# One core, mLSTM and two expert layers: GpSimd's DMAs on two semaphores, an earlier first row load, another order of the weight split, the last block in halves

## The reference, cut to what matters

```python
# layer 1, expert e (exactly 384 tokens):
h = np.maximum(x[mask] @ w1[e], 0.0); out[mask] = h @ w2[e]        # 320 -> 1024 -> 320
# layer 2, expert e (as many tokens as chose it):
h = np.maximum(x[mask] @ w1[e], 0.0)
out[mask] = gate_w[mask, None] * (h @ w2[e])
```

## Time and profile before

| what | value |
|---|---|
| median of 3 runs | 801.45 us (800.43 to 802.65) |
| the profiled execution | 801.36 us, span 799.6 us |
| busy PE, DVE, ACT, POOL | 743.6, 433.1, 315.8, 407.8 us |
| TensorE clock granted, mean | 0.889 of full speed |
| chain that ended last | PE 60%, DVE 10%, POOL 10%, DMA 10%, issue 5%, ACT 2% |

### The profile page before, as it was taken

How to read it: one execution, slowest core, us unless ns; L and a number is a source line. 1 busy time by engine, 2 the same in 40 slices (tenths; PEclk the granted TensorE clock), 3 DMA queues, 4 the chain that set the end, 5 groups by cost and what they waited for, 6 DMA issues and landing times.

```text
span 799.6 us, 21236 instructions
## 1 busy us (share of the span) xinstructions
PE 743.6 (93%) x7388; PEld 649.0 (81%) x7395; DVE 433.1 (54%) x1243; ACT 315.8 (39%) x822; POOL 407.8 (51%) x557
## 2 busy tenths in 40 slices
PE   7999999898899988999999998799999999989992
PEld 3777778677777767999999997489899888979992
DVE  7898887666666674266666666633232332323221
ACT  3666666410000003567766677323233233323320
POOL 4677764700000017787878866507454474465530
PEclk9999999855555557999999999899999999999996
DMA  6666669526722203654644652456576866932310
GB/s 179 206 216 204 188 198 305 166 89 233 240 82 80 82 10 118 188 163 137 195 157 145 199 158 86 141 173 172 170 230 182 237 167 192 275 103 83 119 49 0
DMA packets 63587, 126.23 MB, mean 158 GB/s; under 512 B 14615, under 2 KB 46384, under 8 KB 61970
## 3 DMA queue, kind: packets, MB, share of 16 engines
q1 hardware_dynamic: 44770, 84.19, 33.8%
q0 software_dynamic: 6864, 29.92, 12.0%
q10 hardware_dynamic: 11872, 10.99, 5.2%
HBM read 93.58 MB, written 15.34 MB: 136 GB/s over the span
## 4 chain that ended last, share of the span: by engine, by line
PE 60%; DVE 10%; POOL 10%; DMA 10%; issue 5%; ACT 2%; SPq 0%; ACTq 0%; POOLq 0%
DMA w_hi<-w_raw 9%; PE bank L1662 8%; PE bank L1663 7%; PE bank L1664 7%; PE bank L1621 5%; POOL w_lo L878 3%; PE bank L1698 3%; POOL w_lo L845 3%; PE bank L1701 3%; PE bank L1702 3%; PE bank L1426 3%; PE bank L1499 2%; PE bank L1469 2%; PE bank L1597 2%; PE bank L1707 1%
## 5 line engine op out<-in xcount | busy, mean ns | idle before, releaser
L1662 PE MATMUL bank<-w_hi,hT_hi 128*128 (+1 forms) x440 | 141.3, 321 | 5.4 <-DVE hT_lo L1247 2.9
L1663 PE MATMUL bank<-w_lo,hT_hi 128*128 (+1 forms) x440 | 137.4, 312 | 0.0
L1664 PE MATMUL bank<-w_hi,hT_lo 128*128 (+1 forms) x440 | 137.1, 312 | 0.0
L878 POOL TENSOR_TENSOR w_lo<-w_raw,w_hi 128x320 fp32r<-128x320 f32 x128 | 109.7, 889 | 34.0 <-DMA w_hi<-w_raw 18.8
L845 POOL TENSOR_TENSOR w_lo<-w_raw,w_hi 128x256 fp32r<-128x256 f32 x128 | 95.2, 774 | 56.2 <-DMA w_hi<-w_raw 53.0
L818 POOL DMA_INDIRECT routing_arena<-x_rows,routing_arena x24 | 23.5, 979 | 151.5 <-DVE routing_arena L1235 142.4
L1662 PEld LDWEIGHTS bank<-w_hi,hT_hi 128*128 128x128 f32 x440 | 83.3, 189 | 8.0 <-issue 5.2
L1663 PEld LDWEIGHTS bank<-w_lo,hT_hi 128*128 128x128 f32 x440 | 83.3, 189 | 0.0
L1664 PEld LDWEIGHTS bank<-w_hi,hT_lo 128*128 128x128 f32 x440 | 83.4, 189 | 0.0
L1316 DVE TENSOR_TENSOR xT_lo<-bank,xT_hi 128x256 fp32r<-128x256 f32 x31 | 13.2, 425 | 110.1 <-ACT xT_hi L673 110.1
L687 ACT ACTIVATE hT_hi<-bank 128x512 fp32r<-128x512 f32 x62 | 33.7, 596 | 95.4 <-PE bank L1811 95.4
(11 more groups left out here) (290 smaller groups left out, 1807.4 us busy)
## 6 DMA issues: line engine op xcount, KB each, us to landing
w_raw<-in_moe_w SPq DMA_DIRECT2D x16, 1280.0 KB, 6.8
w_raw<-in_moe_w SPq DMA_DIRECT2D x16, 1024.0 KB
turn_arena<-in_moe_w2t SPq DMA_DIRECT2D x12, 768.0 KB, 4.9
w_raw<-in_moe_w SPq DMA_DIRECT2D x32, 256.0 KB
w_hi<-w_raw POOLq DMA_DIRECT2D x6, 1280.0 KB, 6.1
w_hi<-w_raw POOLq DMA_DIRECT2D x6, 1024.0 KB, 7.8
routing_arena<-x_sorted ACTq DMA_DIRECT2D x31, 160.0 KB
mlstm_arena<-in_q SPq DMA_DIRECT2D x32, 120.0 KB
```

Source lines behind the costliest of these rows:

```text
L878: last = nc.gpsimd.tensor_tensor(w2_part(w2_lo, n)[:, k, :], w2_raw[:, k, :], w2_part(w2_hi, n)[:, k, :], ALU.subtract)
L1662: T.matmul(dst, a_hi, b_hi, start=first, stop=False)
L1663: T.matmul(dst, a_hi, b_lo, start=False, stop=False)
L1664: return T.matmul(dst, a_lo, b_hi, start=False, stop=last)
```

## The change

It puts all DMAs of POOL on two semaphores, `landed_a` and `landed_b`, in place of nine. With one semaphore for several DMAs in flight a count tells which have landed only at the sum of all that were issued on it, so some waits are placed anew: the third gather of the first layer-1 expert is issued after the first has landed, and the output waits at every fourth block for all outputs before it (before, each waited for the one two before it). It makes the first two row loads of layer 2 depend on two numbers (`lead`) that DVE works out from expert 0's count, ahead of the tables; the first block's slot is fixed; 27 idle matmuls in place of 34. In `split_weights` the third slice of w1 is copied first and split first, then slices one and two, each with a DMA of its own, and w2's DMA is issued between the two. The second slice of expert 0's lo part is made by DVE in `logits_copies`. The last block's down product starts after half of its hidden values: PE turns the first half between the two halves of down(29), and down(30) goes to another bank.

```diff
-        scattered = sem("scattered")
+        landed_a, landed_b = sem("landed_a"), sem("landed_b")
-        hi1_ready, hi2_ready = sem("hi1_ready"), sem("hi2_ready")
-        rows_ready = sem("rows_ready")
-        rows_first = [sem(f"rows_first{b}") for b in range(BPE)]
-        stored = [sem(f"stored{s}") for s in range(2)]
...
+        A_FIRST, B_FIRST = 32, 16
+        A_SCATTERED = A_FIRST + 16 * G
+        B_ROWS = B_FIRST + 16 * (G - BPE)
+        A_WEIGHTS, B_WEIGHTS = 64, 16
+        B_STORED = B_ROWS + B_WEIGHTS * (E - RING)
...
-            def hidden_hi(i):
-                act.wait_ge(yb_ready, G + i + 1)
+            def hidden_hi(i, last=False):
                 for f in range(2):
+                    if last and f == 0:
+                        act.wait_ge(pe_made, PED["half_down"])
+                    elif last or f == 0:
+                        act.wait_ge(yb_ready, G + i + 1)
                     act.wait_ge(ht_ready, 2 * i + f + 1 + 2)
                     nc.scalar.activation(hT_hi[:, 4 * f:4 * f + 4, 0:128], bank[3 + f][:, :].rearrange("p (k t) -> p k t", k=4), ACT.Copy).then_inc(hh_ready, 1)
...
-                act.wait_ge(dve_made, DVED["first_rows"])
-                first = [act.value_load(tab2[0:1, 3, i:i + 1], min_val=0, max_val=E * REGION) for i in range(2)]
-
                 act.wait_ge(front_pads, 16 * (E + 1))
-                act.wait_ge(scattered, 16 * G)
+                first = []
+                for i in range(2):
+                    act.wait_ge(dve_made, DVED[f"lead{i}"])
+                    first.append(act.value_load(lead[0:1, i:i + 1], min_val=0, max_val=E * REGION))
+                act.wait_ge(landed_a, A_SCATTERED)
                 for i in range(2):
                     row_loads(first[i], i)
                 x_hi(0, 0)
+                act.wait_ge(dve_made, DVED["first_rows"])
                 next_rows(2, 0)
...
                 for b in range(BPE):
                     j = BPE * e + b
+                    if e == 0 and b == 2:
+                        pool.wait_ge(landed_a, 16)
                     pool.indirect_dma_start(rows[:, b, 0:KT * 128], None, x_sorted[:, :],
-                                            bass.IndirectOffsetOnAxis(ap=order[:, j:j + 1], axis=0)).then_inc(rows_ready if e else rows_first[b], 16)
-
-            def load_hi1(n):
-
-                s, m = n % RING, n - RING
-                pool.wait_ge(raw1_ready, 48 * (n + 1))
-
-                if m >= E:
-                    pool.wait_ge(slot1_free, m - E + 1)
-                pool.dma_start(w1_hi[:, s, 0:2, :], w1_raw[:, 0:2, :]).then_inc(hi1_ready, 16)
-                for h in range(2):
-                    pool.dma_start(w1_hi[64 * h:64 * h + LOW, s, 2, :], w1_raw[64:64 + LOW, 2, :]).then_inc(hi1_ready, 16)
+                                            bass.IndirectOffsetOnAxis(ap=order[:, j:j + 1], axis=0)).then_inc(landed_b if e or b == 1 else landed_a, 16)
 
             def make_lo1(n):
-                s, by_act = n % RING, n < E + RING
-                by_dma = n - E - RING
+                s = n % RING
                 if n:
                     pool.wait_ge(w2_ready, n)
-                if not by_act:
-                    pool.wait_ge(hi1_ready, 48 * (by_dma + 1))
-                for k in range(2):
+                for k in range(2 if n else 1):
                     for h in range(2):
-                        if by_act:
-                            pool.wait_ge(hi1_act, 2 * KT * n + 2 * k + h + 1)
-                        for q in range(2):
-                            c = slice(h * HF + q * HF // 2, h * HF + (q + 1) * HF // 2)
-                            last = nc.gpsimd.tensor_tensor(w1_lo[:, s, k, c], w1_raw[:, k, c], w1_hi[:, s, k, c], ALU.subtract)
-                if by_act:
-                    last.then_inc(w1_ready, 2)
-                    return
-                last.then_inc(w1_ready, 1)
-
-            def make_tail1(n):
+                        pool.wait_ge(hi1_act, 2 * KT * n + 2 * k + h + 1)
+                        last = lo1_half(s, k, h)
+                last.then_inc(w1_ready, 2 if n else 1)
+
+            def lo1_half(s, k, h):
+                for q in range(2):
+                    c = slice(h * HF + q * HF // 2, h * HF + (q + 1) * HF // 2)
+                    last = nc.gpsimd.tensor_tensor(w1_lo[:, s, k, c], w1_raw[:, k, c], w1_hi[:, s, k, c], ALU.subtract)
+                return last
+
+            def make_lo2(n):
                 s = n % RING
-                pool.wait_ge(w1_ready, 2 * n + 1)
-                pool.wait_ge(scattered, 16 * G)
-                pool.wait_ge(rows_ready, 16 * (G - BPE))
+                if n:
+                    pool.wait_ge(w1_ready, 2 * n + 2)
+                for k in range(FT):
+                    pool.wait_ge(hi2_act, FT * n + k + 1)
+                    last = lo2_part(n, k)
+                last.then_inc(w2_ready, 1)
+
+            def lo2_part(n, k):
+                return nc.gpsimd.tensor_tensor(w2_part(w2_lo, n)[:, k, :], w2_raw[:, k, :], w2_part(w2_hi, n)[:, k, :], ALU.subtract)
+
+            def split_weights(n):
+                s, m = n % RING, n - RING
+                at_a, at_b = A_SCATTERED + A_WEIGHTS * (m - E), B_ROWS + B_WEIGHTS * (m - E)
+                pool.wait_ge(raw1_ready, 48 * (n + 1))
+                pool.wait_ge(slot1_free, m - E + 1)
+                pool.wait_ge(w2_ready, n)
+                for h in range(2):
+                    pool.dma_start(w1_hi[64 * h:64 * h + LOW, s, 2, :], w1_raw[64:64 + LOW, 2, :]).then_inc(landed_a, 16)
+                pool.dma_start(w1_hi[:, s, 0, :], w1_raw[:, 0, :]).then_inc(landed_a, 16)
+                pool.dma_start(w1_hi[:, s, 1, :], w1_raw[:, 1, :]).then_inc(landed_b, 16)
+                pool.wait_ge(landed_a, at_a + 48)
                 for h in range(4):
                     c = slice(h * HF // 2, (h + 1) * HF // 2)
                     last = nc.gpsimd.tensor_tensor(w1_hi[64:128, s, 2, c], w1_raw[64:128, 2, c], w1_hi[64:128, s, 2, c], ALU.subtract)
                 last.then_inc(w1_ready, 1)
-
-            def load_hi2(n):
-                s, m = n % RING, n - RING
+                pool.wait_ge(w1_ready, 2 * n + 1)
+                for h in range(2):
+                    lo1_half(s, 0, h)
                 pool.wait_ge(raw2_ready, 16 * (n + 1))
-
-                if m >= E:
-                    pool.wait_ge(slot2_free, m - E + 1)
-                pool.dma_start(w2_part(w2_hi, n), w2_raw[:, :, :]).then_inc(hi2_ready, 16)
-
-            def make_lo2(n):
-                s, by_act = n % RING, n < E + RING
-                by_dma = n - E - RING
-                pool.wait_ge(w1_ready, 2 * n + 2)
-                if not by_act:
-                    pool.wait_ge(hi2_ready, 16 * (by_dma + 1))
+                pool.wait_ge(slot2_free, m - E + 1)
+                pool.dma_start(w2_part(w2_hi, n), w2_raw[:, :, :]).then_inc(landed_a, 16)
+                pool.wait_ge(landed_b, at_b + 16)
+                lo1_half(s, 1, 0)
+                lo1_half(s, 1, 1).then_inc(w1_ready, 1)
+                pool.wait_ge(landed_a, at_a + 64)
                 for k in range(FT):
-                    if by_act:
-                        pool.wait_ge(hi2_act, FT * n + k + 1)
-                    last = nc.gpsimd.tensor_tensor(w2_part(w2_lo, n)[:, k, :], w2_raw[:, k, :], w2_part(w2_hi, n)[:, k, :], ALU.subtract)
+                    last = lo2_part(n, k)
                 last.then_inc(w2_ready, 1)
 
...
+            pool.wait_ge(landed_a, A_SCATTERED)
+            pool.wait_ge(landed_b, B_ROWS)
             for n in range(E + RING, 2 * E):
                 split_weights(n)
...
-                if b > 1:
-                    pool.wait_ge(stored[b % 2], 16 * (b // 2))
+                if b and b % 4 == 0:
+                    pool.wait_ge(landed_b, B_STORED + 16 * b)
                 pool.indirect_dma_start(out, bass.IndirectOffsetOnAxis(ap=ids[:, b:b + 1], axis=0),
-                                        tokens[:, b, 0:DM], None, bounds_check=N - 1, oob_is_err=False).then_inc(stored[b % 2], 16)
-            for s in range(2):
-                pool.wait_ge(stored[s], 16 * ((NB2 + 1 - s) // 2))
+                                        tokens[:, b, 0:DM], None, bounds_check=N - 1, oob_is_err=False).then_inc(landed_b, 16)
+            pool.wait_ge(landed_b, B_STORED + 16 * NB2)
...
+                if g in (G - 6, G - 5):
+                    h = g - (G - 6)
+                    c = slice(h * HF, (h + 1) * HF)
+                    dve.wait_ge(hi1_act, 2 + h + 1)
+                    last = V.tensor_tensor(w1_lo[:, 0, 1, c], w1_raw[:, 1, c], w1_hi[:, 0, 1, c], ALU.subtract)
+                    if h:
+                        last.then_inc(w1_ready, 1)
...
+                done = bank[6 if isinstance(i, int) and i == NB2 - 1 else 5]
...
                         x_lo(i + 1, 1 - s)
+                    else:
+                        hidden_lo(i, (0,))
                     result(i - 1)
```

(49 more changed lines are left out.)

27 lines of the change are left out of this document (12 added, 15 removed).

## The result

The changed kernel took 794.07 us (median of 7, 793.05 to 795.99), the kernel before 801.79 us beside it on the same chip (median of 7, 798.2 to 805.11): ratio 0.9905, 95% interval 0.9879 to 0.993. That is a gain of 7.7 us where 15.3 had been forecast. The profiled execution took 794.07 us, with a span of 792.3 against 799.6. Single executions that came out some per cent longer at a lower granted clock, whatever the kernel, are left out of all ratios.

What follows compares the result with a forecast made beforehand. The prediction took PE to set the pace, POOL's weights nearly late in layer 2, and the span to end on POOL's DRAIN. Its six steps summed to -15.3 us: 801.4 to 786.1 us, whole range 783.8 to 793.5.

Steps and rivals of the forecast that it cites:

- Step 6: POOL's closing DRAIN of 8.48 us: seven semaphores fewer at 0.88 us each shorten it; -6.1 us, bounds 0 and -6.6.
- Rival (a): The closing DRAIN doesn't care about semaphores, being fixed or by DMAs issued; the rest holds, 792.2 us; chance 0.27.
- Step 1: Expert 0's second lo slice on DVE: first-phase `keys` lines run faster without POOL beside them; -1.2 us, bounds 0 and -1.6.
- Step 2: Layer 1's first expert: the third gather waits for the first to land; +0.7 us, bounds 0.3 and 1.2.
- Step 3: Start of layer 2: the first row loads go out earlier; -0.7 us, gain 0.4 to 1.4 or 0.
- Step 4: Layer 2's weight split: POOL's wait for w1's copies falls 2.1 us per turn, ending PE's stall at block 23; -4.6 us.
- Step 5: Last block in halves: no PE idle ahead of down(30), clock stays up; -3.4 us, bounds -1.8 and -3.6.

## Why the prediction was wrong, step by step

**Step 6, the DRAIN, failed: +0.5 us measured, -6.1 forecast.** The prediction read the right row, and said that what the DRAIN does isn't shown; then it chose the semaphores, "since no other row of the trace gives a reason" and since the number of DMAs "hardly changes". But the row and a count would have allowed both, and the second forecast was as easy: 103 DMAs make 8.4 us, and six more make 0.5 us more. One sample can't choose between two counts; the mistake was to put 6.1 us, the largest term of the sum, on that choice with a chance of 0.50 against 0.27. What the runs show in its place is 82 ns for each DMA since the last DRAIN, with two, three, nine or ten semaphores. The prediction had named this sign of being wrong itself: "if the DRAIN grew". Rival (a), in its form "by DMAs issued", is what happened: 792.2 us, plus 0.5 for six DMAs which it named and didn't price.

**The other steps** sum to -9.2 in the forecast. The trace has -9.8 from the logits to the last result, +0.6 of it in layer 1 in no step; then the mLSTM stage adds 2.1. That the two come so near is luck in part: 1.35 us of blocks 0 to 22 are not shown to be the change's, and some 1.5 us each at block 23 and at the last block were falls of the granted clock in the one trace of the kernel before.

- *Step 1*, -1.2 forecast, -1.6 + 0.45 found. `keys` gained all of its bound. The new pair on DVE cost the path nothing that shows, as costed; but DVE's own pair L1079 went from 1.96 to 2.50 us and its cover ran out (PE then waited 0.38 us). Its first instruction begins 0.17 us after one of GpSimd's now and takes 1229 ns; in the earlier trace rows it begins 0.01 us before one and takes 690. The Trainium skill (SBUF — State Buffer, Who interferes with whom) says that a DVE instruction with two SBUF inputs and a GpSimd one that reads SBUF shut each other out for a whole instruction. The trace agrees, for the pair that had not moved. Beside the new one (1082 and 671 ns) two of GpSimd's lo instructions took 1170 and 1306 ns in place of some 725.
- *Step 2*, +0.7 forecast, +0.8 found. *Step 3*, -0.7 forecast, -0.7 found to the first row load, and 0.35 more up to the first turn.
- *Step 4*, -4.6 forecast, -4.15 found at block 23. Each wait fell by 2.8 us (17.0 over six), not by 2.1, and w1 of n = 15 was whole at 704.1 (705 forecast). What the stall is worth differs between traces of the old split: 4.15 us here, with a wait of 2.53 us and a granted clock of 0.50 from 711.4 to 714.7 us behind it, and 1.3 us in the kernel before with three DRAINs, with a wait of 1.03 us and the clock at 1.00. The other 1.35 us, of blocks 0 to 22, are in no step and not shown to be the change's: that stretch took between 187.2 and 192.4 us in sixteen traces (190.3 before, 188.9 after), with no wait for weights above 0.3 us in it. By the Trainium skill (DMA: Bandwidth & Descriptors, Anatomy of one DMA) the bytes saved are worth an estimated 1.2 us per wait; the trace shows more than twice that. The prediction set all traced waits far above that rule's 5.6 us for the three copies; two of the six were 5.9 and 7.1 us.
- *Step 5*, -3.4 forecast, -3.5 found, of which about 1.5 is the clock. The prediction's bound of -1.8 was near the part that is sure (2.0), but for another reason: it let the clock fall in the changed kernel too, while in the runs it is the idle of 1.8 us that did not always bring a fall.
- *The start*, +2.1 us, was in no step, and is no effect of the change. Granted clock of PE, the first two stretches of 20 us, of before, of after and of the kernel with thirty DMAs (stretch, length, PE busy, PEclk, DMA share, GB/s):

```profile
0.00:20.00 20.00, 15.03 (x89) 1.00 0.63 179
20.00:40.00 20.00, 19.68 (x320) 1.00 0.66 206
```

```profile
0.00:20.00 20.00, 14.38 (x69) 0.91 0.61 174
20.00:40.00 20.00, 20.00 (x295) 1.00 0.63 194
```

```profile
0.00:20.00 20.00, 15.40 (x93) 1.00 0.64 179
20.00:40.00 20.00, 18.35 (x168) 0.65 0.47 154
```

The stage's last scan on DVE started at 128.6 to 128.7 us in the three traces whose clock was 1.00 in both stretches (before, and the changed kernel with three DRAINs and with the pair on GpSimd again), at 129.6 to 130.8 in the twelve at 0.91 to 0.95 in the first stretch, and at 139.1 in the last one shown. None of these kernels differs from another in that stage, and the kernel before with three DRAINs, whose edit comes into play only behind 500 us, is one of the twelve (0.91, 130.15). So 1 to 2 us of the 794.07 us, as far as traces of one execution each can tell, are the spread of a start that the change has nothing to do with. Whether a build always starts the same way no run shows.

The measured 794.07 lies 0.6 us outside the range, which went to 793.5: its upper end was taken at (a) with small change, and held neither the DRAIN's growth nor a start at the lower clock.

## What to carry to other kernels

A row that occurs once can be divided by anything; before a term is built on such a quotient, count the other candidates too, and price the forecast by each. Where GpSimd issues many DMAs, look at its closing DRAIN: here it cost 82 ns for each since the last DRAIN, and DRAINs put where GpSimd idles anyway took 8.8 us of it out of the span. And a wait for part of a transfer, then work on that part, can be worth much the same whichever part is first: here the six waits came to 36.0 and 33.2 us, against 53.0 for all of it.

## What the runs showed of the hardware that was not expected

- GpSimd's DRAIN: 44 ns and 82 ns for each DMA it has issued since the last DRAIN, most of them long landed, 1 to 119 of them; the same price for the 48 gathers and scatters together (3.93 us) as for 30 plain copies (2517 ns). No price for semaphores. With 134 and 149 in all it stayed at 8974 ns.
- The granted clock doesn't always fall behind the same idle: 1.79 us ahead of down(30) left the matmuls at 5.3 us in one trace and at 3.8 in two others.
- The first 40 us can run below the full clock, and cost 1 to 2 us, once 10, in kernels whose first 40 us are the same.
